# Decayed linear attention: the states over five chunks by one scan on VectorE in place of four dependent steps

## The reference

```python
# q, k, v, alpha: (4, 8, 768, 48) fp32
for t in range(S):
    state = alpha[:, :, t, :, None] * state + einsum('bhd,bhe->bhde', k[:, :, t], v[:, :, t])
    y[:, :, t] = einsum('bhd,bhde->bhe', q[:, :, t], state)
x = y.transpose(0, 2, 1, 3).reshape(3072, 384)
x = moe(x)     # 8 experts, top 1, 384 -> 1024 -> 384, relu, times the gate
out = (elu(x @ w_in) @ w_out)     # 384 -> 2048 -> 384
```

## Time and profile before

| what | value |
|---|---|
| median of 3 runs | 904.02 us (901.72 to 905.69) |
| the profiled execution, its own time | 905.82 us |
| its span in the profile | 904.2 us |
| PE busy (TensorE) | 873.4 us, 97% |
| DVE busy (VectorE) | 435.5 us, 48% |
| ACT busy (ScalarE) | 321.8 us, 36% |
| POOL busy (GpSimd) | 283.8 us, 31% |
| attention | about the first 175 us of the span |

### The profile page before, as it was taken

How to read it: one execution, slowest core, us unless ns; L and a number is a source line. 1 busy time by engine, 2 the same in 40 slices (tenths; PEclk the granted TensorE clock), 3 DMA queues, 4 the chain that set the end, 5 groups by cost and what they waited for, 6 DMA issues and landing times. The chain is left out here.

```text
span 904.2 us, 16339 instructions
## 1 busy us (share of the span) xinstructions
PE 873.4 (97%) x5725; PEld 780.5 (86%) x5725; DVE 435.5 (48%) x828; ACT 321.8 (36%) x709; POOL 283.8 (31%) x279
## 2 busy tenths in 40 slices
PE   7999998889999999999999999999999999999994
PEld 5888887778898998998988999999999999999894
DVE  7889899662223223222224545445445445445442
ACT  4576665523222323222222233223223223223221
POOL 3235665355635674375617102001001001001001
PEclk9999999799999999999999999999999999999998
DMA  9977775668877878747617002002002002000000
GB/s 154 171 133 142 163 156 151 226 218 288 255 244 247 289 252 255 253 118 222 177 53 228 18 0 71 1 1 71 1 1 70 1 1 70 1 1 36 1 1 35
DMA packets 140975, 107.92 MB, mean 119 GB/s; under 512 B 103354, under 2 KB 129074, under 8 KB 140898
## 3 DMA queue, kind: packets, MB, share of 16 engines
q0 software_dynamic: 25696, 66.09, 23.0%
q1 hardware_dynamic: 115202, 40.79, 20.3%
HBM read 89.51 MB, written 17.35 MB: 118 GB/s over the span
## 5 line engine op out<-in xcount | busy, mean ns | idle before, releaser
L1427 POOL DMA_INDIRECT out<-of,idi x24 | 23.6, 983 | 370.1 <-DVE of L1513 305.4
L1247 PE MATMUL bank<-WX,hdTh 128*128 (+1 forms) x496 | 130.7, 345 | 3.0 <-DVE hdTl L1300 1.7
L1471 PE MATMUL bank<-xT_h,wi_h 128*128 128x512 f32 x288 | 114.2, 396 | 0.0
L1471 PE MATMUL bank<-xT_l,wi_h 128*128 128x512 f32 x288 | 113.6, 395 | 0.0
L1471 PE MATMUL bank<-xT_h,wi_l 128*128 128x512 f32 x288 | 113.4, 394 | 0.0
L1531 ACT ACTIVATE ee<-bank 128x512 f32<-128x512 f32 x96 | 57.3, 597 | 148.7 <-PE bank L1471 144.8
L1553 DVE TENSOR_SCALAR em<-ee 128x512 f32<-128x512 f32 x96 | 43.1, 449 | 136.6 <-ACT ee L1531 134.4
L1233 PE MATMUL bank<-WX,xdTh 128*128 (+1 forms) x372 | 99.6, 403 | 2.9 <-ACT xdTh L1273 1.4
L1534 ACT ACTIVATE g_h<-gg 128x512 fp32r<-128x512 f32 x96 | 60.6, 631 | 114.2 <-DVE gg L1558 112.5
L1171 POOL TENSOR_TENSOR WX<-raw_w,WX 128x3072 fp32r<-128x3072 f32 x14 | 95.7, 6834 | 15.4 <-DMA WX<-moe_w 11.4
L1562 DVE TENSOR_TENSOR g_l<-gg,g_h 128x512 fp32r<-128x512 f32 x96 | 69.4, 722 | 60.2 <-ACT g_h L1534 59.3
(11 more groups left out here) (215 smaller groups left out, 1444.1 us busy)
## 6 DMA issues: line engine op xcount, KB each, us to landing
WX<-moe_w POOLq DMA_DIRECT2D x14, 1536.0 KB, 10.0
raw_w<-moe_w POOLq DMA_DIRECT2D x14, 1536.0 KB, 8.1
xd<-sorted_x SPq DMA_DIRECT2D x31, 193.0 KB, 5.1
sorted_y<-yd SPq DMA_DIRECT2D x31, 192.5 KB, 4.3
xg<-sorted_y SPq DMA_DIRECT2D x6, 770.0 KB, 4.4
nat_a<-alpha SPq DMA_DIRECT2D x32, 144.0 KB, 3.4
nat_k<-k SPq DMA_DIRECT2D x32, 144.0 KB, 3.3
nat_q<-q SPq DMA_DIRECT2D x32, 144.0 KB, 4.4
```

Source lines behind the costliest of these rows:

```text
L1247: last = pe.matmul(y_out(t)[:, 0:DM], hdT[a][:, k * P:(k + 1) * P], WX[:, bass.ds(off + (b * WE + KD * F + k * DM), DM)], start=(k == 0 an ...
L1471: last = pe.matmul(bank[4 + i % 2][:, :], a[:, k, w], b[:, k, :], start=(k == 0 and m == 0), stop=(k == KD - 1 and m == 2))
```

## The change

What it does, in the attention alone:

- `st` and `std` are laid out [partition, 48, 5]: the five chunks of one column lie side by side, so that the state of a chunk has its 48 elements 5 elements (20 bytes) apart. State 1 goes to `st` like the others.
- A new table `carry` (two buffers, 128 x 240 fp32) holds gam(2) to gam(5) repeated for all 48 columns, with a zero at the first of every five. GpSimd zeroes both tables once at the start and then fills one for each pair in a new step `Gz` (line 1048 of the changed kernel), which stands between `M1` and `Za`.
- VectorE runs one scan of 240 elements in place of the four steps, out(j) = out(j-1) * carry(j) + st(j); the zeros restart it at each column. Its step keeps the name `S5`.
- `Ys0` and `Ys1` both wait for `S5`, and load their weights from `std` with the 20-byte step. `St` no longer waits for `Ys1` of two pairs before, and `Gm` no longer for `S5` of two pairs before, but `Gz` does.

```diff
+        carry = [at(f"carry{u}", [P, D, C - 1], where=a_at) for u in range(2)]
...
-        st = [at(f"st{u}", [P, C, D], where=a_at) for u in range(2)]
-        std = [at(f"std{u}", [P, C, D], where=a_at) for u in range(2)]
+        st = [at(f"st{u}", [P, D, C - 1], where=a_at) for u in range(2)]
+        std = [at(f"std{u}", [P, D, C - 1], where=a_at) for u in range(2)]
...
-                    ("S2", 0), ("S3", 0), ("S4", 0), ("S5", 0))
+                    ("S5", 0))
...
-        ROUND_PO = (("Gm", 1), ("M1", 0), ("Za", 2), ("Zm", 2))
+        ROUND_PO = (("Gm", 1), ("M1", 0), ("Gz", 1), ("Za", 2), ("Zm", 2))
...
+            for t in carry:
+                po.memset(t[:, :, :], 0.0)
             po.memset(resets[:, :, :], 1.0).then_inc(s_c0, 1)
...
-                    acA.wait(pe, "St1", n)
-                    veA.wait(pe, "S5" if i else "S2", n)
+                    veA.wait(pe, "S5", n)
...
-                            last = pe.matmul(y_bank(n, i)[rows, m * P:(m + 1) * P], std[u][rows, c, :],
+                            last = pe.matmul(y_bank(n, i)[rows, m * P:(m + 1) * P], std[u][rows, :, c - 1],
...
                     acA.wait(ve, f"St{i}", n)
-                    veA.wait(ve, f"S{i - 1}", n)
+                    poA.wait(ve, "Gz", n)
                     peA.wait(ve, "Ys1", n - 2)
-                    return ve.scalar_tensor_tensor(out=std[u][:, i, :], in0=std[u][:, i - 1, :], scalar=gam[u][:, i:i + 1],
-                                                   in1=st[u][:, i, :], op0=ALU.mult, op1=ALU.add)
+                    return ve.tensor_tensor_scan(flat(std[u]), flat(carry[u]), flat(st[u]), 0.0, ALU.mult, ALU.add)
...
-                    peA.wait(ac, "Ys1", n - 2)
                     veA.wait(ac, "S5", n - 2)
-                    return ac.activation((st if i > 1 else std)[u][:, i, :], bank[5][:, (i - 1) * D:i * D], ACT.Copy,
+                    return ac.activation(st[u][:, :, i - 1], bank[5][:, (i - 1) * D:i * D], ACT.Copy,
...
+                if name == "Gz":
+                    poA.wait(po, "Gm", n)
+                    veA.wait(po, "S5", n - 2)
+                    return po.tensor_copy(carry[u][:, :, 1:], gam[u][:, 2:].unsqueeze(1).to_broadcast([P, D, C - 2]))
                 veA.wait(po, "G", n)
-                veA.wait(po, "S5", n - 2)
+                poA.wait(po, "Gz", n - 2)
```

More of the change, by code:

```diff
@@ L336, in steps_ve @@
             out_ = with_route(ROUND_VE, ROUTE_VE, n)
-            sums = [(f"S{i}", n) for i in range(2, C)]
+            sums = [("S5", n)]
             if n == PAIRS - 1:
```

## The result

Over 20 runs of each kernel the changed one took 905.20 us in the median (903.36 to 908.61), the one before 902.94 us (900.68 to 906.08). The ratio is **1.0026**, 95% interval 1.0015 to 1.0038: a little slower, and within the 0.5% that counts as no change. The predicted 907.0 against 904.02 was a ratio of 1.0033. The two intervals don't meet, so a set of runs differs from another by more than either interval tells.

What follows compares the result with a forecast made beforehand. The prediction took TensorE to bound the attention's rounds, with VectorE counting only by when it releases Ys. Its terms, 1.8 us for plain rounds and 1.2 for round 8, made +3.0 us: 907.0 against 904.02, range 901 to 916.

Steps and rivals of the forecast that it cites:

- The scan and its start: VectorE, plain round: scan takes 0.66 us, starts at St1 + 1.08 after all five St, ends 0.20 us earlier than the chain.
- the 0.5 forecast: VectorE's idle time ahead of the scan was to grow by some 0.5 us a round.
- +0.23 us a plain round: TensorE: all of Ys starts after the scan, so KT comes 0.23 us later; eight rounds, +1.8 us.
- the zero for the 20-byte step: Strided weight loads and ScalarE's writes taken to cost 0; upper ends 3 us for loads with cover, 1.5 us for ScalarE.
- The strided loads: TensorE's Ys loads: at most 37 ns each, some 27 hidden; the rival had them show, 8 us, 915 in all, chance 0.22.
- `Gz` in plain rounds: GpSimd's copy of 192 elements, 343 ns: GpSimd has the time in plain rounds, and meeting scan F is covered.
- +1.2 us in round 8: Gz delays GpSimd's scatters, the suf scan catches the second, and TensorE waits longer for mask M1: +1.2 us.
- the rest follow 1 to 1.2 us late: Scatters behind the caught second one, and round 8's mask M1 behind them, were to come 1 to 1.2 us late.
- Rounds 0, 1, 7, 12 to 15 together zero: Rounds with VectorE or GpSimd late anyway: each between -0.7 and +0.23 us, taken as 0 together; round 12 also 0.
- that fall goes away: Rival: TensorE's clock stays up after round 14's wait, saving 5.1 us, 902 in all; chance 0.08.

Runs made afterwards that it cites:

- no_gz: The changed kernel without the copy Gz, so the scan reads zeros and no state is carried on: 909.48 us, ratio 1.0039.
- after_again: The changed kernel once more, unaltered, on another set of runs: 910.06 us, ratio 1.0060 against the kernel before.
- psum_early: The changed kernel with the scan reading KV from PSUM (24-byte step), without the St steps, between Qh0 and Qh1: 900.58 us, ratio 0.9941.
- steps_only: The kernel before with only the changed layout of st and std (20-byte step), all instructions and waits kept: 908.47 us, ratio 1.0032.
- before_late: The kernel before with the last three scatters of a batch moved behind Zm: 908.79 us, ratio 1.0028.
- psum_late: The changed kernel with the scan straight from PSUM, no St steps, and the last three scatters behind Zm: 897.48 us, ratio 0.9911.
- psum_late2: Scan straight from PSUM, no St steps, last three scatters behind Zm, repeated on another set of runs: 896.68 us, ratio 0.9938.
- psum_end: The changed kernel with the scan straight from PSUM and no St steps, scan placed behind Qh1, scatters not moved: 898.07 us, ratio 0.9949.

## Why the prediction was right, and where its sum was not

The forecast was +3.0 us, within 0.5%; the ratio 1.0026 is 2.3 us. The total is near, but partly by luck: its terms were off by +0.95, -1.2 and -1.5 us, and these errors offset each other in part.

- **The scan and its start: right.** 0.657 us against 0.66. It starts 1.14 to 1.15 us behind `St1`, against 1.08. In plain rounds nothing of the shorter work reached TensorE, and it turned into waiting for ScalarE, as the step on its start had it: that wait ahead of the states grew from 5.7 to 13.7 us, 8.0 us, and 7.9 us of work were saved (17.7 less 9.8). All idle time there grew from 10.5 to 13.9 us, 0.23 us a round and not the 0.5 forecast.
- **+0.23 us a plain round: the mechanism right, the size too small.** It is 0.34, +2.75 us in eight rounds where I had 1.8. The step that failed is the zero for the 20-byte step: 0.05 us is the last `St`'s end (1.11 against 1.06), and another 0.04 to 0.05 is `Ys` to `KT` (1.26 against 1.22). Also round 10 was a poor base: its `St1` to `KT` is 2.79, that of rounds 2 to 4 is 2.75.
- **The strided loads: the bound was right, the rival wrong.** I had at most 37 ns a load and 27 of them hidden. No row then had the step; VectorE's copies were the nearest. A load became 37 ns longer (159 against 122), and 33 of these were hidden: 20 loads take 1.12 us, before 1.04. That is 0.7 us in 16 rounds, not the rival's 8. A rule of the Trainium skill ("Advanced Engine Details and Errata", "Memory Cachelines") has a step past the line of 16 bytes cost something. The trace agrees for loads, for ScalarE's writes (305 to 353 ns) and for VectorE (286 to 308), and shows how little of it reaches the path. Five writes of `st`, each 48 ns longer, end only 0.05 us later, since they overlap and just the last one's length counts. Their 48 ns are above the bound of 37 that I had taken.
- **`Gz` in plain rounds: right,** by `no_gz`.
- **+1.2 us in round 8: wrong.** It was +0.03. Here is GpSimd in the changed kernel, then VectorE's scans and TensorE's wait:

```profile
88.44 1.25 POOL L1036 DMA_INDIRECT sorted_x<-xb,slot  x1 [0.18 <-DVE LR L853]
89.99 2.40 POOL L1036 DMA_INDIRECT sorted_x<-xb,slot  x1 [0.30 <-issue]
...
94.06 0.99 POOL L1036 DMA_INDIRECT sorted_x<-xb,slot  x1 [0.17 <-issue]
95.35 1.64 POOL L1036 DMA_INDIRECT sorted_x<-xb,slot  x1 [0.30 <-issue]
...
98.27 0.88 POOL L1028 TENSOR_SCALAR_AFFINE_SELECT asb<-asb 128x768 f32<-128x768 f32 x1
```

```profile
89.89 1.73 DVE L858 TENSOR_TENSOR_SCAN suf<-al,seedG 128x768 f32<-128x768 f32 x1
...
94.47 1.76 DVE L866 TENSOR_TENSOR_SCAN inv<-al,seedF 128x768 f32<-128x768 f32 x1
```

```profile
99.20 0.86 PE L665 MATMUL bank<-asb,vn 128*48 128x128 f32 x12 [0.72 <-POOL asb L1028]
```

The second scatter was caught, as predicted, and ended at 92.39, 0.77 us after the scan. But `Gz` was not what made it late: `Gz` ran from 86.16, `F` from 86.20 for 1.90 us in place of 1.76, and the first scatter came 0.34 us behind the end of `F`, as before (88.10 and 88.44, 86.35 and 86.69). What changed is that the `suf` scan came 1.79 us behind the end of `F`, before 2.34. But the step "the rest follow 1 to 1.2 us late" did not hold. The fourth started at 94.06, 0.41 us ahead of the next scan, and got through in 0.99 us. The fifth was caught, and ended 0.76 us after that scan, as whatever is caught in it would have. A caught scatter's end hangs on the scan's, so lateness ahead of it is absorbed, and TensorE waited the same 0.72 us. In `after_again` the scatters fell in the same way, the fourth at 93.95 and the scan at 94.35, and yet round 8 was 0.97 us longer; TensorE waited 1.20 us there for ScalarE's eviction of `A`, so that length isn't the scatters catching a scan.
- **Rounds 0, 1, 7, 12 to 15 together zero: wrong by 1.5 us,** and this hid the missing part above. Two rounds, 14 and 15, give back 1.56. In round 14 the step had `Ys1` at its old time; but there VectorE is late, its shorter work reaches TensorE almost whole (0.67 us, the -0.7 that I had as the lower end), and another 0.67 us is the clock that fell later. The rest, 0.22 us, is round 15. My rival "that fall goes away" had the place, but its whole 5.1 us did not come in this profile.

Terms of the sum against what the profiled pair shows: 1.8 and 2.75; 1.2 and 0.03; 0 and -1.56, together 3.0 and 1.2, and 2.3 by the ratio. The 1.1 us between the last two are a profiled execution of each kernel against medians.

Open stays what holds ScalarE and TensorE up in rounds 8 and 12. The scatters' transfers run at the same time (DMA share 1.06 of the stretch in `psum_early`, where the mask behind the scatters was late), and moving three scatters changed which rounds are long, so they are my suspicion; but no run took the traffic away, and it isn't shown. Open too is what lets the clock stay up: it fell in `before` after 1.95 us of idle time, and in `steps_only` after 1.99 and in `before_late` after 1.96 it did not.

## What to carry to other kernels

A chain of small steps may be slow and still cost little, because it runs along with its producer and lets its consumer start on the first result. Before four steps become one scan, ask what the scan must wait for and who could use the first of the four; here that cost 0.34 us a plain round although the scan is 0.7 us shorter. Where VectorE was late anyway, in round 14, the shorter scan did pay. The gain came only when the scan took its input from where TensorE had left it, so that the wait and ScalarE's five steps went together: 0.9% and 0.6% below the kernel before in two sets, with the last scatters behind `Zm`. And where a delay is predicted to pass on, look for the next long wait on its way, which may absorb it, as the next scan did with the late scatters.

## What the runs showed of the hardware that I had not expected

- A 20-byte step makes a load of 48 columns 37 to 39 ns longer and a ScalarE write of 48 elements 48 ns longer, but in a row of them the spacing grows by just 4 ns a load (1.12 us for 20 against 1.04).
- Matmuls that write PSUM with a 24-byte step take as long as even ones: 0.79 us for 20 passes in both.
- An indirect DMA on GpSimd that started inside a VectorE scan of 768 elements ended 0.76 or 0.77 us after the scan, in each of the four cases looked at; one that started 0.41 us ahead of the scan took its usual 0.99 us.
- TensorE's half clock after round 14 lasted 10.2 us before and 6.8 us in the changed kernel. In `steps_only`, `before_late` and the four `psum` runs from `psum_late` on the granted clock stayed 1.00 through the attention's last rounds, and round 15 was 7.29 to 9.15 us in place of 11.07. In `psum_late2` and `psum_end` it fell in the first expert tiles instead (means of 0.52 at 172 to 174 us and 0.50 at 174 to 176).
